# Second mixture of experts: routing list order, early expert counts, warm-up lengths, the drain between experts, and weights waited for in halves

## The reference, cut to what matters

```python
def _moe2_ref(x, w_skip, w_gate, w1, w2):      # x: 1536 x 512, E = 8, F = 1024
    do_compute = (x @ w_skip) > 0
    out = x.copy()
    xc = x[do_compute]
    logits = xc @ w_gate
    e_idx = np.argmax(logits, axis=1)
    probs = softmax(logits); gate_w = probs[arange, e_idx]
    for e in range(E):
        mask = e_idx == e
        h = np.maximum(xc[mask] @ w1[e], 0.0)
        y[mask] = gate_w[mask, None] * (h @ w2[e])
    out[do_compute] = xc + y
```

## Time and profile before

| what | value |
|---|---|
| median of 3 runs | 733.49 us (730.63 to 738.72) |
| the profiled execution's own time | 731.53 us |
| its span, first to last instruction | 729.7 us |
| busy: PE, DVE, ACT, POOL | 652.2, 379.0, 292.8, 204.7 us |
| attention and first routing | to about 139 us |
| first mixture | from about 151 to 473 us |
| second routing | to about 520 us |
| second mixture | from about 526 to 718 us, and the last scatter |

### The profile page before, as it was taken

One profiled execution on the slowest core, in us unless ns is written; L12 is line 12 of the kernel. 1 busy time (PEld: TensorE's weight loads), 2 busy tenths in 40 slices (PEclk: granted clock), 3 DMA queues, 4 the chain that ended last, 5 costly groups with the idle time before them and its releaser, 6 DMA issues.

```text
span 729.7 us, 13727 instructions
## 1 busy us (share of the span) xinstructions
PE 652.2 (89%) x4168; PEld 575.2 (79%) x4168; DVE 379.0 (52%) x761; ACT 292.8 (40%) x503; POOL 204.7 (28%) x227
## 2 busy tenths in 40 slices
PE   5697883799999999999999999999599979999793
PEld 4576763489999999999999999876487768777682
DVE  2676687535363545454453636403565476745721
ACT  2365662034352434443432435214155455645520
POOL 1538670220232405060413324030112222222220
PEclk9899997599999999999999999999799999999997
DMA  9999996126182727456371927167175587556221
GB/s 196 203 232 235 269 301 198 37 60 230 49 234 71 213 79 166 158 113 212 72 252 48 251 72 220 58 141 242 24 245 151 156 288 236 161 161 232 42 42 16
DMA packets 94866, 116.14 MB, mean 159 GB/s; under 512 B 55940, under 2 KB 56068, under 8 KB 94800
## 3 DMA queue, kind: packets, MB, share of 16 engines
q1 hardware_dynamic: 77264, 90.83, 41.9%
q0 software_dynamic: 10464, 23.81, 15.9%
q10 hardware_dynamic: 7072, 0.70, 0.7%
HBM read 100.01 MB, written 20.18 MB: 165 GB/s over the span
## 4 chain that ended last, share of the span: by engine, by line
PE 71%; SPq 8%; DMA 6%; DVE 6%; issue 5%; ACT 1%; POOL 1%; POOLq 0%; DVEq 0%; ACTq 0%
PE bank L788 20%; PE bank L794 20%; PE bank L893 15%; SPq L499 5%; DMA xg<-x_moe,ix_take 2%; PE bank L777 2%; SPq L514 2%; DMA out<-y_sb,ix_put 2%; PE bank L766 2%; PE bank L645 2%; PE bank L695 1%; PE bank L717 1%; PE bank L909 1%; DVE col_val L1580 1%; PE bank L678 1%
## 5 line engine op out<-in xcount | busy, mean ns | idle before, releaser
L1454 DVE TENSOR_TENSOR w_lo<-stage,w_hi x120 | 141.6, 1221 | 21.7 <-ACT w_hi L1018 19.5
L1018 ACT CAST w_hi<-stage x120 | 119.6, 1047 | 9.8 <-PEq L935 9.7
L788 PE MATMUL bank<-tok_hi,w_hi 128*128 128x416 f32 x256 | 91.3, 357 | 1.8 <-DVE tok_lo L1636 1.8
L794 PE MATMUL bank<-unit_hi,w_hi 128*128 128x416 f32 x256 | 92.5, 361 | 0.0
L788 PE MATMUL bank<-tok_hi,w_lo 128*128 128x416 f32 x256 | 90.5, 354 | 0.0
L794 PE MATMUL bank<-unit_lo,w_hi 128*128 128x416 f32 x256 | 90.2, 352 | 0.0
L794 PE MATMUL bank<-unit_hi,w_lo 128*128 128x416 f32 x256 | 89.6, 350 | 0.0
L1670 DVE SCALAR_TENSOR_TENSOR unit_lo<-bank,unit_hi 128x416 fp32r<-128x416 f32 x64 | 37.8, 591 | 98.2 <-ACT unit_hi L1104 98.2
L1104 ACT ACTIVATE unit_hi<-bank 128x416 fp32r<-128x416 f32 x64 | 33.2, 519 | 130.7 <-PE bank L788 130.7
L1304 POOL DMA_INDIRECT x_moe<-rows_out,ix_put x32 | 58.7, 1835 | 53.2 <-DVE rows_out L1659 45.9
L788 PE MATMUL bank<-tok_lo,w_hi 128*128 128x416 f32 x256 | 58.7, 350 | 0.0
(11 more groups left out here) (162 smaller groups left out, 1106.1 us busy)
## 6 DMA issues: line engine op xcount, KB each, us to landing
stage<-in_moe_w SPq DMA_DIRECT2D x128, 512.0 KB, 5.6
v_win<-in_v SPq DMA_DIRECT2D x24, 192.0 KB, 6.8
x_moe<-rows_out SPq DMA_DIRECT2D x12, 260.0 KB, 3.3
x_att<-x_sb POOLq DMA_DIRECT2D x12, 256.0 KB, 5.2
x_sb<-x_moe SPq DMA_DIRECT2D x12, 256.0 KB, 2.8
out<-x_moe SPq DMA_DIRECT2D x4, 768.0 KB, 8.6
late_raw<-in_v SPq DMA_DIRECT2D x6, 384.0 KB, 6.9
stage<-in_k SPq DMA_DIRECT2D x6, 256.0 KB, 6.7
```

Of the source, the lines that this page charges most:

```text
L788: last = eng.matmul(ps_unit[f % 2][:, 0:W], w, x, start=(i == 0), stop=(i == len(mine) - 1))
L794: last = eng.matmul(ps_out[chunk][:, 0:W], w[:, WC // 2 + f, chunk * P:(chunk + 1) * P], h[:, f % UNITS, :], start=(f == 0 and i == 0), st ...
L1018: eng.copy(piece(w_hi[n % SETS], j), stage[:, j, :]).then_inc(s_hi, 1)
L1454: eng.tensor_tensor(piece(w_lo[n % SETS], j), stage[:, j, :], piece(w_hi[n % SETS], j).bitcast(F32), ALU.subtract)\
```

## The change

The routing's counts come out earlier: `totals` (the count, and the number of rounds or blocks) is moved out of `index_lists` to stand before the one-hot matrices of the last tiles, and counts a new semaphore `s_counted`; PE and ACT wait for that instead of `s_route`, and POOL waits for it, loads its counts, and waits for `s_listed` last. In `index_lists` the empty slots are marked after `take_ix`. The second routing takes the largest logit with one reduction in place of one search per tile, and finds the expert by a comparison, an addition and a smallest value in place of an index search per tile. The first group's `lists` are moved behind the loop over tiles. The unread products before the first gathered tokens are 24 in place of 26 in the first mixture, with 4 more behind each of the four parts' transposes, and 24 in place of 14 in the second. The drain behind each expert of the second mixture is gone; ACT waits instead for the count that PE's last product of a slot raises. PE waits for four of an expert's eight pieces at its start, and for all eight before the products by w2.

```diff
@@ PE, first_mixture
-                eng.wait_ge(s_route, 1)
+                eng.wait_ge(s_counted, 1)
                 eng.reg_load(counts, todo_i[0:1, 0:E])
                 eng.wait_ge(s_first, PIECES // 2)
-                keep_warm(26, ps_turn)
+                keep_warm(24, ps_turn)
                 for t in range(PARTS):
                     eng.wait_ge(s_take[t], 16)
                     turn_x(0, t, ps_out[t])
+                    keep_warm(4, ps_turn)
@@ PE, second_mixture
+                eng.sem_inc(S["y"], 1)
-                eng.wait_ge(s_route, m + 1)
+                eng.wait_ge(s_counted, m + 1)
                 eng.reg_load(counts, todo_i[0:1, 0:E])
-                keep_warm(14, ps_y)
+                keep_warm(24, ps_y)
...
-                    eng.wait_ge(s_lo, PIECES * n)
+                    eng.wait_ge(s_lo, PIECES * n - PIECES // 2)
...
                         eng.wait_ge(S["hth"], sv * 2 + 1)
+                        eng.wait_ge(s_lo, PIECES * n)
                         eng.wait_ge(S["ye"], sv + 1)
                         products(ps_y, down, 0, T // 2)
...
-                    eng.drain().then_inc(s_wfree, 1)
@@ PE, second routing
                 if t == first[1] + 3:
                     ranks(1, first)
-                if t == first[1] + 5:
-                    lists(1, first)
+            lists(1, first)
             ranks(1, second)
             lists(1, second)
@@ ACT, second_mixture (and s_counted for s_route in both mixtures)
                     if E + 1 < n < 2 * E:
-                        eng.wait_ge(s_wfree, n - 1 - E)
+                        eng.wait_ge(S["y"], eng.snap(slot, min_val=0, max_val=2 * NT + E) + 1)
+                        eng.sem_inc(S["set"], 1)
@@ POOL, both mixtures
-                eng.wait_ge(s_listed, 2)
-                eng.wait_ge(s_gates, 16 * sum(len(GROUPS[i]) for i in range(m + 1)))
-                eng.reg_load(counts, todo_i[0:1, 0:E])
+                eng.wait_ge(s_counted, 2)
+                eng.reg_load(counts, todo_i[0:1, 0:E])
+                eng.wait_ge(s_gates, 16 * sum(len(GROUPS[i]) for i in range(m + 1)))
+                eng.wait_ge(s_listed, 2)
@@ DVE
+            def totals(m):
+                then(eng.tensor_copy(count[:], ps_rank[:, NT * E:(NT + 1) * E]))
+                if m == 0:
+                    ...                       # rounds: three instructions, as before
+                else:
+                    then(eng.tensor_scalar(count_i[:], count[:], float(P - 1), None, ALU.add))
+                    then(eng.tensor_scalar(todo_i[:], count_i[:], 7, None, ALU.arith_shift_right))
+                eng.sem_inc(s_counted, 1)
@@ DVE, route: second routing
+                    then(eng.tensor_reduce(top[:, tiles, 0], ranked[:, tiles, 0:E], AX.X, ALU.max))
...
+                    names = c("share")
+                    then(eng.tensor_tensor(below[:, tiles], ranked[:, tiles, 0:E],
+                                           wide(top[:, tiles, 0:1], [P, T, E]), ALU.is_lt))
+                    then(eng.tensor_tensor(below[:, tiles], below[:, tiles],
+                                           wide(names.rearrange(...), [P, T, E]), ALU.add))
+                    then(eng.tensor_reduce(top_f[:, 0, tiles], below[:, tiles], AX.X, ALU.min))
...
+                if t1 == NT:
+                    totals(m)
                 for t in range(t0, t1):
@@ DVE, index_lists: the counts are gone, and
+                eng.wait_ge(s_list, (2, 3)[m] * NT)
+                then(eng.tensor_copy(take_ix[:], numbers))
+                eng.sem_inc(s_listed, 1)
                 then(eng.tensor_tensor(empty[:], ...))
                 then(eng.tensor_scalar(empty[:], empty[:], c("spare"), None, ALU.mult))
-                eng.wait_ge(s_list, (2, 3)[m] * NT)
-                then(eng.tensor_copy(take_ix[:], numbers))
-                eng.sem_inc(s_listed, 1)
                 then(eng.tensor_tensor(put_ix[:], numbers, empty[:], ALU.add))
                 eng.sem_inc(s_route, 1)
@@ DVE, second_mixture
-                        eng.wait_ge(S["y"], sv + 1)
+                        eng.wait_ge(S["y"], sv + 2)
```

More of the change, by code:

```diff
@@ L118, in constants @@
     parts["expert"] = np.tile(np.arange(E, dtype=np.float32), (P, 1))
+    parts["share"] = np.tile(np.arange(E, dtype=np.float32) / (2 * E), (P, 1))
     parts["column"] = np.tile(np.arange(NCOL, dtype=np.float32), (P, 1))
@@ L268, in build @@
         top_e = sb_in(routing, "top_e", [P, NT, E])
+        below = sb_in(routing, "below", [P, NT, E])
         hot = sb_in(routing, "hot", [P, 2, NT, E])
@@ L349, in build @@
         s_listed = sem("s_listed")
+        s_counted = sem("s_counted")
         s_route = sem("s_route")
@@ L382, in build @@
             "hte": "DVE: the rest is in ht_lo",
-            "y": "PE: the expert's output",
+            "y": "PE: the expert's output (one more than slots)",
             "ix": "DVE: the slot's destinations are in ix_put",
+            "set": "ACT: one more set of weights is free",
             "ye": "DVE: the output is in y_sb (one more than slots)",
@@ L1478, in by_tile @@
                 return wide(a[:, t0:t1].rearrange("p (t o) -> p t o", o=1), shape)
+            def totals(m):
+                then(eng.tensor_copy(count[:], ps_rank[:, NT * E:(NT + 1) * E]))
+                if m == 0:
+                    then(eng.tensor_tensor(
+                        more[:], wide(count[:].rearrange("p (e o) -> p e o", o=1), [P, E, ROUNDS]),
+                        wide(c("round").rearrange("p (o r) -> p o r", o=1), [P, E, ROUNDS]), ALU.is_gt))
+                    then(eng.tensor_reduce(todo_f[:], more[:], AX.X, ALU.add))
+                    then(eng.tensor_copy(todo_i[:], todo_f[:]))
+                else:
+                    then(eng.tensor_scalar(count_i[:], count[:], float(P - 1), None, ALU.add))
+                    then(eng.tensor_scalar(todo_i[:], count_i[:], 7, None, ALU.arith_shift_right))
+                eng.sem_inc(s_counted, 1)
             def route(m, group):
@@ L1499, in route @@
                     ranked = logit2
[L1500 to L1504, removed]
+                if m == 0:
+                    for t in range(t0, t1):
+                        last = eng.max(top[:, t, :], ranked[:, t, 0:E])
+                    then(last)
+                    for t in range(t0, t1):
+                        last = eng.max_index(top_ix[:, t, :], top[:, t, :], ranked[:, t, 0:E])
+                else:
+                    then(eng.tensor_reduce(top[:, tiles, 0], ranked[:, tiles, 0:E], AX.X, ALU.max))
                 eng.tensor_tensor(top_d[:, tiles, :], ranked[:, tiles, 0:E],
@@ L1530, in route @@
                        .then_inc(s_mask, 1)
-                    then(eng.scalar_tensor_tensor(first_f[:, 0, tiles], top_f[:, 0, tiles], float(NBLK),
-                                                  away[:, tiles], ALU.mult, ALU.add))
+                    then(eng.scalar_tensor_tensor(first_f[:, 0, tiles], top_f[:, 0, tiles],
+                                                  float(2 * E * NBLK), away[:, tiles], ALU.mult, ALU.add))
                 eng.wait_ge(s_tope, number)
@@ L1584, in index_lists @@
             def index_lists(m):
[L1585 to L1594, removed]
+                eng.wait_ge(s_list, (2, 3)[m] * NT)
+                numbers = ps_list[:, 0:NCOL].rearrange("p (e n) -> p e n", e=E)
+                then(eng.tensor_copy(take_ix[:], numbers))
+                eng.sem_inc(s_listed, 1)
                 then(eng.tensor_tensor(
```

18 lines of the change are left out of this document (11 added, 7 removed).

## The result

The changed kernel takes 726.5 us, the median of 14 runs (723.39 to 731.26), against 733.89 us before (14 runs). The ratio is 0.9894, with a 95% interval of 0.9871 to 0.9918, or 7.8 us less (6.0 to 9.5); the two medians are 7.4 apart. The forecast was 9.1 us less. The profiled execution has a span of 724.9 us, 4.8 less than that of before. Its attention part happens to be late: the last activation before the first routing starts at 119.50, against 118.14. This 1.36 us has nothing to do with the change, and I take stretches from such a point on and not from zero.

A forecast was written before the change was run, and what follows sets the result against it. The prediction took POOL's rounds, as slow as PE, to bound the second mixture. First routing 2.2, second routing 0.8 and second mixture 6.1 us sum to 9.1 us less, median 724.4 us, from 720.4 to 728.3.

The forecast's parts named there:

- POOL's rounds bound the second mixture: Second mixture: POOL's gather and scatter rounds, 13.93 us each against PE's slot of 12.66, limit what PE's savings bring.
- all of it comes back: Rival, second mixture: POOL's round falls to 12.24 us, drains and weights give 14.2 us, kernel 716.3 us; chance 0.12.
- PE was to wait for gathers in several slots: Sign, second mixture: PE's transposes of tokens wait for POOL in several slots, in place of idle PE at expert ends.
- The term of 6.1 us: Second mixture: of 14.2 us from drains and weights, all that PE can come forward before the last slot's gathered tokens.
- First routing and unread products: First routing and mixture: earlier start 0.4 us, full clock for the first real products 1.8; together 2.2 us gained.
- without the pause the clock stays up: First mixture: with PE not pausing before the real products, the first 24 take 4.54 us in place of 6.33.
- Second routing: Second routing: gather 3.0 us and unread products 3.5 us earlier, but ten more products leave 0.8 us gained.
- Drains: Expert ends in the second mixture: five open gaps of 0.6 us on PE go, 3.0 us.
- Weights in halves: Second mixture: PE's two waits for weights, 3.8 and 4.0 us, go, and with them the slow clocks, 3.2 us.
- A wait of 2 us for DVE in that expert: Sign that the prediction is wrong: such a wait on PE in the expert after a one-block one.
- The rival in which DVE takes the place of the second stall: Slot behind a one-block expert: DVE's late queue keeps that stall, 3.6 us left in all, 729.9 us; chance 0.18 with another case.
- The sum: Whole kernel: 2.2 + 0.8 + 6.1 = 9.1 us less, median 724.4 us.

The follow-up runs named there:

- the variant with 14: Changed kernel with 14 unread products before the second mixture in place of 24; ratio 0.9885 to the kernel before.

## Why the prediction was right, and where it was off

**POOL's rounds bound the second mixture.** Right, and the main point. The round was to stay near 13.9 us and did, at 13.83; PE came forward until it waited for the last slot's gather (0.72 us at 695.63). With the rounds out of the way the edits on PE give 15.0 us of the mixture (191.4 to 176.4) in place of 4.4. The rival "all of it comes back" had the round fall by itself. It did not, but its 14.2 us were about the right price of what was hidden (its own terms, 3.0, 7.8 and 3.2, make 14.0). The way by which the rounds hold PE was only partly foreseen. PE was to wait for gathers in several slots and waited 0.9 us for them in all; the larger part, 5.9 us, came through the scatters, for which DVE waited before it emptied the output. That it is POOL and not DVE's own work shows in the variant with both transfers in flight, where these waits are gone.

**The term of 6.1 us was too large.** I took it from the last gather and PE's turning of those tokens, as all that PE could come forward. PE did come 7.1 us forward. But the last output also hangs on POOL: its scaling waits until the scatter before has landed, and that stands behind one more gather that nobody needs. DVE waited 3.06 us there, and the mixture gained 4.4 us. In the other variants that POOL bounds, and that differ from the changed kernel only elsewhere (drain, lists, unread products), it took 186.7 to 189.8 us, so the term is 2 to 5 us. Most of that spread is the length of POOL's rounds, 13.80 to 14.09 us, for which the prediction had allowed 3 us either way.

**First routing and unread products.** The term was 2.2 us. By traces, up to the end of the first 24 real products, it was 0.7 (39.54 to 38.86) in the profiled execution and 0.6 to 2.2 in the variants, all with 24 products and four behind each part. The unread products started 0.9 us earlier (1.4 forecast), and the time of 24 of them, by when the clock rises, decides the rest: 7.1 to 8.6 us, where I had 7.2 to 8.2. The step "without the pause the clock stays up" was right for this kernel, but as a gain over the kernel before it leans on a fall that doesn't always happen.

**Second routing.** Counted from the eleventh tile's logits (505.94 before, 506.50 after), the gather is 2.2 us earlier (3.0 forecast), the unread products 3.0 (3.5 forecast), and the first product 0.65 (0.8 forecast). PE turned the first tokens 1 to 2 us after they had landed (2 to 3 forecast). In the other variants with 24 unread products and the lists behind the loop, the first product came from 0.8 us earlier to 0.6 later, as these products took 7.15 to 8.52 us. That ten more unread products spend what the routing gives was shown by the variant with 14.

**Drains.** Forecast 3.0 us for PE, taken up by POOL's slack; measured nothing beyond POOL's rounds in the changed kernel, and 4.0 without POOL's bound, for the two that stood under the waits for weights are open then.

**Weights in halves.** The first wait never held, nor the second. DVE's lateness behind the one-block expert was there, 1.36 us for `ht_lo` (1.5 forecast). In the next slot, the second of the same expert, PE waited 2.01 us more, for DVE to empty the output, which had waited for the scatter of 8.46 us. A wait of 2 us for DVE in that expert was one of the signs by which the prediction called itself wrong, and it came. It did not cost what that sign stood for: DVE's own queue was not the bound, POOL's rounds were, and both waits are gone with POOL's transfers together. The rival in which DVE takes the place of the second stall did not come; PE ran through that slot.

**The sum.** In the two profiled executions, from the last activation before the first routing to the end, 0.7, 0.65 and 4.4 and some 0.4 elsewhere make 6.2 us, where 9.1 had been forecast; the measured 7.8 has an interval of 6.0 to 9.5. The forecast of 724.4 us lies 2.1 us under the median. The mechanism was right, and two of its three terms were too large.

## What to carry to other kernels

When two engines are each nearly the bound, price what is taken from one by the other's room, and look for that room at the last item too, output and all: here the edits on PE shortened the second mixture by 4.4 us alone (2 to 5 in other executions), the one on POOL by 0.2 alone, and both by 15.2. An engine that issues a transfer, waits for its landing, issues the next and waits again has a round of two latencies; if the two don't depend on each other, issue both and wait afterwards. Unread products to keep a clock up must be counted against what they delay, and over more than one run.

## What the runs showed of the hardware

- A scatter of 128 rows that adds took 3.6 to 5.9 us from issue to landing before (median 4.8), and up to 8.5 in the changed kernel (median 5.0), beside loads of weights. This is the stretch of the 8.46 us, with the DMA engines 0.96 busy:

```profile
601.90:610.40 8.50, 7.63 (x35) 5.84 (x34) 5.20 (x6) 4.99 (x7) 2.57 (x1) 1.00 0.96 312
```

- PE's clock stayed at 2.4 GHz over a pause of 1.51 us in one run and fell to 1.2 GHz after pauses of 1.79 us in two others, with the granted clock at 0.58 in the first 2 us of the products of one (151 to 153) and 0.51 from 156 to 157 in the other. But in the changed kernel it stayed at 2.4 GHz over the longer pause of 2.01 us that ends at 611.54, so the length of a pause alone did not decide it:

```profile
611.00:612.00 1.00, 0.46 (x2) 0.45 (x3) 0.56 (x2) 0.00 (x0) 0.18 (x1) 1.00 0.98 379
612.00:613.00 1.00, 1.00 (x6) 0.74 (x5) 0.69 (x1) 0.00 (x0) 0.53 (x1) 1.00 0.28 107
```

- 24 unread products took from 7.06 to 8.57 us in the same place of the program, by when the clock rose in their course.
- The same attention code ended up to 7.5 us apart (the activation before the first routing at 117.19 to 124.66 us), in profiled executions of kernels that don't differ before it. A change of 1 us can't be seen in the whole time beside that.
